# The x products of a head moved behind the projections, and its weighted sum cut into four runs

## The reference

```python
# attention, 2 x 8 heads, 768 tokens, head_dim 64, 6 hash bits
q_bits = einsum(q, proj) > 0;  k_bits = einsum(k, proj) > 0
mask = bucket(q_bits)[:, None] == bucket(k_bits)[None, :]
scores = where(mask, q @ k.T / 8, -1e9)
attn = exp(scores - max) / (sum + 1e-9)
x = (attn @ v) laid out as [1536 tokens, 512]
# experts with a capacity: a token takes its best open expert
logits = x @ w_gate                      # [1536, 8]
# greedy over all (token, expert) by falling logit, 192 tokens an expert
out[mask_e] = relu(x[mask_e] @ w1[e]) @ w2[e]
# dense layer on all tokens
h = x @ w_in;  out = (h * sigmoid(h)) @ w_out
```

## Time and profile before

| what | value |
|---|---|
| median of 3 runs | 798.89 us (794.78 to 799.8) |
| profiled execution, time | 797.15 us |
| profiled execution, span from first to last instruction | 795.4 us |
| mean granted TensorE clock | 0.99 |
| PE busy over the span | 753.1 us (95%) |
| VectorE busy | 475.0 us (60%) |
| ScalarE busy | 270.5 us (34%) |
| GpSimd busy | 155.9 us (20%) |

### The profile page before, as it was taken

How to read it: one execution, slowest core, us unless ns; L and a number is a source line. 1 busy time by engine, 2 the same in 40 slices (tenths; PEclk the granted TensorE clock), 3 DMA queues, 4 the chain that set the end, 5 groups by cost and what they waited for, 6 DMA issues and landing times.

```text
span 795.4 us, 19347 instructions
## 1 busy us (share of the span) xinstructions
PE 753.1 (95%) x7772; PEld 634.3 (80%) x7777; DVE 475.0 (60%) x1097; ACT 270.5 (34%) x551; POOL 155.9 (20%) x193
## 2 busy tenths in 40 slices
PE   8899999999998899999999999999999999999996
PEld 4577777677776658999999999988887888878885
DVE  4877777777776788977977942463333432333321
ACT  4777667766774401221222212321013111220111
POOL 5523644545434100100100100000002000020001
PEclk9999999999997999999999999999999999999999
DMA  7165354553632034534544647710001000010001
GB/s 157 35 149 126 77 136 108 126 124 80 155 105 68 23 112 142 199 147 133 187 160 133 228 144 247 264 46 1 1 0 54 0 0 0 0 53 0 0 0 53
DMA packets 58194, 75.07 MB, mean 94 GB/s; under 512 B 28736, under 2 KB 43072, under 8 KB 57120
## 3 DMA queue, kind: packets, MB, share of 16 engines
q1 hardware_dynamic: 54592, 67.12, 29.4%
q0 software_dynamic: 2208, 7.21, 2.8%
q10 hardware_dynamic: 1344, 0.04, 0.1%
HBM read 64.92 MB, written 6.29 MB: 90 GB/s over the span
## 4 chain that ended last, share of the span: by engine, by line
PE 80%; issue 8%; ACT 4%; DVE 4%; DMA 2%; POOL 1%; DVEq 0%; ACTq 0%; SPq 0%; POOLq 0%
PE quad_ps L1535 17%; PE quad_ps L1424 10%; PE quad_ps L1436 10%; PE quad_ps L1264 9%; PE score_ps L1518 8%; PE quad_ps L1518 7%; PE score_ps L1249 5%; PE score_ps L1250 3%; PE work_ps L1366 2%; ACT k_bits L531 2%; PE pv_ps L1234 2%; PE work_ps L1234 2%; DMA area<-x_rows,ids_now 1%; PE quad_ps L1273 1%; ACT att_area L537 1%
## 5 line engine op out<-in xcount | busy, mean ns | idle before, releaser
L1535 PE MATMUL quad_ps<-y_s,w_in_s 128*128 128x512 f32 x576 | 137.8, 390 | 2.7 <-DVE y_s L1171 2.0
L885 DVE TENSOR_SCALAR_CACHE_REDUCE att_area<-score_ps 128x768 f32<-128x768 f32 x96 | 91.9, 958 | 64.7 <-PE score_ps L1250 63.4
L1535 PEld LDWEIGHTS quad_ps<-y_s,w_in_s 128*128 128x128 f32 x576 | 107.9, 188 | 26.2 <-DVE y_s L1171 2.8
L1189 DVE TENSOR_TENSOR gate<-quad_ps,sig 128x512 f32<-128x512 f32 x48 | 33.2, 692 | 146.4 <-ACT sig L671 146.4
L537 ACT ACTIVATE att_area<-att_area 128x768 f32<-128x768 f32 x96 | 90.0, 938 | 75.1 <-DVE att_area L885 74.2
L671 ACT ACTIVATE sig<-quad_ps 128x512 f32<-128x512 f32 x48 | 28.7, 598 | 210.6 <-PE quad_ps L1535 210.6
L1424 PE MATMUL quad_ps<-area,experts_w 128*128 128x192 f32 x512 | 96.1, 334 | 1.5 <-ACT area L631 1.2
L1436 PE MATMUL quad_ps<-area,experts_w 128*128 128x192 f32 x512 | 87.2, 328 | 0.0
L1249 PE MATMUL score_ps<-k_parts,q_parts 128*128 128x512 f32 x192 | 73.7, 384 | 12.7 <-DVE att_area L885 11.6
L1424 PEld LDWEIGHTS quad_ps<-area,experts_w 128*128 128x128 f32 x512 | 81.8, 190 | 2.1 <-ACT area L631 2.1
L1436 PEld LDWEIGHTS quad_ps<-area,experts_w 128*128 128x128 f32 x512 | 82.9, 190 | 0.0
(11 more groups left out here) (202 smaller groups left out, 1094.2 us busy)
## 6 DMA issues: line engine op xcount, KB each, us to landing
experts_w<-in_moe_w SPq DMA_DIRECT2D x16, 2048.0 KB, 9.8
att_area<-in_v SPq DMA_DIRECT2D x64, 192.0 KB, 3.8
experts_w<-in_moe_w_in SPq DMA_DIRECT2D x8, 512.0 KB, 5.5
w_out_raw<-in_moe_w_out SPq DMA_DIRECT2D x4, 1024.0 KB, 8.9
experts_w<-in_k SPq DMA_DIRECT2D x16, 192.0 KB, 3.3
experts_w<-in_q SPq DMA_DIRECT2D x16, 192.0 KB, 3.6
k_bits<-k_parts SPq DMA_DIRECT2D x16, 192.0 KB, 3.5
x_rows<-att_area SPq DMA_DIRECT2D x8, 384.0 KB, 3.1
```

Source lines behind the costliest of these rows:

```text
L885: nc.vector.tensor_scalar(probs[c % 3], score_ps[0][:, 0:S], 0.5 * BIG, None, ALU.min, ALU.min, accum_out=neg_max[:, c:c + 1]).then_inc(s_ ...
L1189: nc.vector.tensor_tensor(gate[:, :], layer_ps[f % 2][:, 0:GT], sig[:, :], ALU.mult).then_inc(s_mul, 1)
L1535: done = nc.tensor.matmul(layer_ps[f % 2][:, 0:GT], w_in_s[:, a, w_cols], y_s[:, c, b, :], start=(c == 0 and a + b == 0), stop=(c == DC - ...
```

## The change

In the new version the x products are no fill any more. They have a semaphore of their own (`s_x_full`), a function of their own on PE (`x_rows`), and always the bank `work_ps`; they come in the third step (t = 2) of a head instead of at the end of the second. The four fills of hash bits, which stood three in the first step and one in the second, stand two and two. A fill's bank is now given by its half. The weighted sum has the shares `[4, 4, 0, 12, 4, 0]`, four runs over five steps, and its part of a step stands between the two fills of that step. The copy of the sums (`turned`) moves from t = 4 to t = 5, and VectorE's drain of x from t = 2 to t = 3. In the last pair, where steps have no fills, two matmuls of 512 columns whose product nobody reads are added in each of the steps 4 and 5 of its first head and 0 and 1 of its second. The number of matmuls that compute something is the same.

```diff
         def events(p, first, last):
-            bits = [] if last and p else [("k_bits", 0, 1), ("k_bits", 1, 1), ("q_bits", 0, 1), ("q_bits", 1, 1)]
-            x = [] if first else [("x", 0, 0)]
-            rows = [] if last else [("k", 0, 2), ("k", 1, 2), ("q", 0, 2), ("q", 1, 2)]
-            at_t = {0: bits[0:3], 1: bits[3:4] + x, 4: rows[0:2], 5: rows[2:4]}
...
+            e = {t: [] for t in range(T)}
+            if not (last and p):
+                e[0], e[1] = [("k_bits", 0, 1), ("k_bits", 1, 1)], [("q_bits", 0, 1), ("q_bits", 1, 1)]
+            if not last:
+                e[4], e[5] = [("k", 0, 2), ("k", 1, 2)], [("q", 0, 2), ("q", 1, 2)]
             return e
...
# ScalarE, pair
-                        if t == 4 and not (first and p == 0):
+                        if t == T - 1 and not (first and p == 0):
                             if not first:
-                                act.wait_ge(s_work_full, w)
+                                act.wait_ge(s_x_full, 2 * g + p - 1)
                             turned(2 * g + p - 1)
...
# VectorE, pair
-                        if t == 2 and not first:
+                        if t == 3 and not first:
                             if p == 0:
                                 dve.wait_ge(s_xw, 16 * g)
                             dve.wait_ge(s_logits, h - 1)
                             dve.wait_ge(s_norm_step, 2 * (h - 1))
-                            i = len(ev[0]) + len(ev[1]) - 1
-                            drain_x(w + i, p, bank_of(first, p, i))
+                            drain_x(h - 2, p, work_banks[0])
...
# TensorE
+            def x_rows(h, bank, free=None):
+
+                rhs = to_x[:, h % H, :] if isinstance(h, int) else to_x[:, bass.ds(h % H, 1), :].rearrange("p a e -> p (a e)")
+                if free is not None:
+                    pe.wait_ge(s_work_free, free)
+                pe.wait_ge(s_turned, h + 1)
+                for t in range(T):
+                    last = nc.tensor.matmul(bank[:, t * DE:(t + 1) * DE], weighted_t[:, t * P:(t + 1) * P], rhs, start=True, stop=True)
+                last.then_inc(s_x_full, 1)
...
-            SHARE = [0, 0, 12, 12, 0, 0]
+            SHARE = [4, 4, 0, 12, 4, 0]
...
-                        for kind, half, i, ahead in ev[t]:
-                            if kind == "x":
-                                fill_work(kind, half, u - 1, h - 2, p, bank_of(first, p, i))
-                            else:
-                                fill_work(kind, half, u if kind == "k" and half == 0 and not first else u - 1, h + ahead,
-                                          (p + ahead) % 2, bank_of(first, p, i),
-                                          x_free=h if kind == "k" and half == 1 and not first else None)
-                                u = u + 1
+                        for slot, (kind, half, ahead) in enumerate(ev[t]):
+                            if slot == 1:
+                                weighted_part(h, p, t, first, g)
+                            fill_work(kind, half, u - 1, h + ahead, (p + ahead) % 2, work_banks[half],
+                                      x_free=h if kind == "k" and half == 0 and not first else None)
+                            u = u + 1
+                        if t == 2 and not first:
+                            x_rows(h - 2, work_banks[0], u - 1)
                         if last and p == 1 and t == T - 2:
                             row_of_first_batch(u)
-                        if not (first and p == 0):
-                            weighted(h - 1, 1 - p, sum(SHARE[0:t]), SHARE[t], g if p else g - 1)
+                        if len(ev[t]) < 2:
+                            weighted_part(h, p, t, first, g)
+                        if last and (p == 0 and t >= T - 2 or p == 1 and t < 2):
+                            keep_busy(2, work_banks[1])
```

More of the change, by code:

```diff
@@ L248, in routed_layers @@
         s_halves = sem("halves_ready")
+        s_x_full = sem("x_ready")
         s_x_free = sem("x_drained")
@@ L385, in k_drained @@
             return PREP * h + 2
-        def bank_of(first, p, i):
-            return work_banks[(i + (p == 1 and not first)) % 2]
         def scatter(pool, G):
@@ L520, in _, with drain_work @@
             nc.scalar.activation(q_nat[0][:, :, 0:D].bitcast(f32r), q_nat[0][:, :, D:P], ACT.Copy).then_inc(s_first_high, 1)
-            def drain_work(kind, half, w, p_next, bank):
+            def drain_work(kind, half, w, p_next):
+                bank = first_banks[w % 4] if isinstance(w, int) and w < PREP else work_banks[half]
                 cols = slice(half * HALF, (half + 1) * HALF)
@@ L550, in _ @@
                 for half in range(2):
-                    i = PREP + 2 * t + half
-                    drain_work("q" if t else "k", half, i, 1, work_banks[i % 2])
+                    drain_work("q" if t else "k", half, PREP + 2 * t + half, 1)
             act.wait_ge(s_halves, 5)
@@ L570, in pair @@
                         n = 2 * T * g + c
-                        if t == 4 and not (first and p == 0):
+                        if t == T - 1 and not (first and p == 0):
                             if not first:
-                                act.wait_ge(s_work_full, w)
+                                act.wait_ge(s_x_full, 2 * g + p - 1)
                             turned(2 * g + p - 1)
-                        for slot, (kind, half_, i, ahead) in enumerate(ev[t]):
+                        for slot, (kind, half_, ahead) in enumerate(ev[t]):
                             if slot == 1:
                                 next_exp(n, c, last)
-                            if kind != "x":
-                                drain_work(kind, half_, w, (p + ahead) % 2, bank_of(first, p, i))
+                            drain_work(kind, half_, w, (p + ahead) % 2)
                             w = w + 1
@@ L959, in pair @@
             def pair(g, first, last):
-                w = work_base(g)
                 for p in range(2):
                     h = 2 * g + p
-                    ev = events(p, first, last)
                     for t in range(T):
@@ L983, in pair @@
                             dve.wait_ge(s_norm_step, 2 * (h - 1))
-                            i = len(ev[0]) + len(ev[1]) - 1
-                            drain_x(w + i, p, bank_of(first, p, i))
-                    w = w + sum(len(ev[t]) for t in range(T))
+                            drain_x(h - 2, p, work_banks[0])
             pair(0, True, False)
@@ L1229, in fill_work @@
                                             start=False, stop=True)
-                else:
-                    rhs = to_x[:, h % H, :] if isinstance(h, int) else to_x[:, bass.ds(h % H, 1), :].rearrange("p a e -> p (a e)")
-                    pe.wait_ge(s_turned, h + 1)
-                    for t in range(T):
-                        last = nc.tensor.matmul(bank[:, t * DE:(t + 1) * DE], weighted_t[:, t * P:(t + 1) * P], rhs,
-                                                start=True, stop=True)
-                last.then_inc(s_work_full, 1)
+                last.then_inc(s_work_full, 1)
+            def x_rows(h, bank, free=None):
[6 more added lines that the diff above has]
+                last.then_inc(s_x_full, 1)
             def scores(c, h, n, crossed):
```

33 lines of the change are left out of this document (13 added, 20 removed).

## The result

| | before | after |
|---|---|---|
| median | 798.76 us (794.78 to 799.8, 4 runs) | 776.67 us (773.34 to 778.48, 4 runs) |
| profiled execution, time and span | 797.15, 795.4 us | 777.72, 775.9 us |

The ratio is 0.9728, with an interval of 0.9679 to 0.9776: 2.7% faster.

The account below looks back on a forecast made before the run. PE's uneven load was taken as the bound: some steps overfull, others at the ring's 2.02 us. Gains of 16.8 (twelve heads), 0.5 (heads 0 and 1) and 4.6 (last pair, net) sum to 21.9, giving 776 us, range 771 to 781.

Parts of the forecast that it names:

- The prices of PE's work: PE's cost per piece, from its starts: score tile 0.70 to 0.81 us, x products 1.35, four blocks 0.93 with following cost.
- The 12 heads: Heads 2 to 13: each 1.40 us shorter, 14.44 us by its six steps, so 16.8 us in all.
- rival 1: ScalarE's copy and drains, 0.4 us margin at step 0's second bits fill, become PE's wait: 782 us; chance 0.10.
- Where the gain lies: In a head: blocks move from long steps to steps with idle PE, and a run precedes the fill that waited.
- The ring's 2.0: One score buffer: VectorE reads it 0.96 us, PE refills it 1.0, plus hand-overs; a step takes at least 2.02 us.
- The last pair: Head 14 to the last score tile: clock stays up (4.1 us), 26.90 becomes 20.9, 6.0 less; net 4.6 after the end's loss.
- The tail: Last score tile to the x products: four blocks behind the turned row, then the copy; 4.90 becomes 6.3, 1.4 us lost.
- Heads 0 and 1: The first two heads, without x products: a gain set at 0.5 us for both, between 0 and 1.4.
- rival 4: Loads become the bound: k or q land late, PE waits in step 4 of every second head; 802 at 15 us; chance 0.04.
- GpSimd's waits stay under 1 us: Sign that the loads are not the bound: GpSimd waits less than 1 us for k and q.
- the 11.2 allowed: Time from the start of v's loads to GpSimd getting k: 11.2 us allowed, 10.6 before the change, 0.6 to spare.

Follow-up runs that it names:

- the run with the blocks in one: The changed kernel with the last head's sixteen blocks, before in two runs (twelve and four), in one run in its fourth step: 776.79 us.
- the kernel with five runs: The changed kernel with the shares 4, 4, 0, 8, 4, 4, the last run in step 5 between the fills of q: 782.73 us.
- the two-input form: The changed kernel with VectorE's small operation on the row sums (adds 1e-9) written with two tensor inputs, same result: 777.04 us.

## Why the prediction held, point by point

The forecast was a gain of 21.9 us from the profiled execution. The medians lie 22.1 apart, the spans of the two profiled executions 19.5. The parts missed by 2.3, 0.5, 0.7 and 0.3 us, the largest because the clock fell in head 0 of one execution and not of the other. So the mechanism and its size held; that the median came within a microsecond is in part luck.

- **The prices of PE's work** held. A run of four was set at 0.93 with the way in; 0.10 in and 0.83 out are measured. Forecast steps of 2.53, 2.42, 2.05, 3.01, 2.46 and 1.97 stand against 2.53, 2.43, 1.96, 3.00, 2.37 and 2.00. The x products cost 1.26 (109.83 to 111.09) and not 1.35; they no longer follow a pause, and a first matmul behind one took 0.11 more; step 4's run and fill cost 0.1 less.
- **The 12 heads** gave 16.3 for 16.8, by two errors that nearly cancel. At 14.29 a head they would give 18.6. The odd heads gave back 1.9 of it (1.0 in head 5, 0.2 in each of four others) with VectorE's hold, which the prediction did not have, and head 2 another 0.4, where GpSimd waited 2.2 us for k.
- **ScalarE's drains** (rival 1, margin 0.4) never showed as a wait of PE. The run between the fills is what hides them: with it behind the fills PE stands 0.29 us in step 0, and with no run there 0.5 to 0.6 us in each of two steps.
- **Where the gain lies** was half seen. The prediction put it down to a more even load of PE, and saw one such wait filled, ahead of the x products. But by its own prices steps 0 and 1 of the kernel before hold 1.8 and 2.4 us of PE's work (a score tile and three fills; a score tile, a fill and x) and took 2.44 and 3.32: about 1.5 us of these "full" steps were waits and the pauses around them. By the same way of summing, the new placement with the old shares should take 15.3 a head, and takes 15.81; the missing 0.5 are the two drains (2.24 and 2.26 instead of 2.0 each). The ring's 2.0 holds for a step with two fills only if the drains are not late.
- **The last pair.** Its clock was sized at 4.1, and 3.8 are measured by the unread products in the old kernel. That the clock stays up was right; that unread products are needed for it was not. The four steps with unread products take 2.02 to 2.07, where three were set at 2.24 and one at 1.97.
- **The tail** lost 1.1 us up to the x products (1.4 forecast), and the run with the blocks in one did not settle whether the blocks or ScalarE's order have it. The other 0.5 us lie between the x products and the dense layer (258.99 us before, 259.54 after); the dense layer takes 270.7 to 270.8 in every profile. That stretch goes with the clock: 257.6 to 258.4 us in the three profiles without a fall in it, 259.0 in the kernel before with 3.4 us at 1.2 GHz, 259.5 to 260.4 in the eight with 6.8, the changed kernel among them, and 260.7 in the two with 10.2. So these 0.5 us need no cause in the change.
- **Heads 0 and 1**, +0.5 forecast and -1.3 measured: the clock fell in head 0 of the profiled execution. Three executions with the same work in head 0 and no fall had it at 12.68 to 12.70, against 13.04 before. In two of them heads 0 and 1 together took 26.97 and 27.00 us against 27.57, so 0.6 less: there the forecast was right.
- **The loads** (rival 4) cost no more than that 0.4 in head 2, though the sign "GpSimd's waits stay under 1 us" failed twice (2.2 in head 2, 1.1 in head 4). In head 2 GpSimd got k 11.50 us behind the start of v's loads, 0.3 over the 11.2 allowed, and the head is 0.4 longer; in head 4 it was 10.4, and nothing was lost. With the end of the sum a step later, in the kernel with five runs, the margin is used up: PE waits for GpSimd's k five times.

## What to carry to other kernels

Look for the places where the bounding engine waits between two of its own instructions, and put movable work exactly there: here twelve blocks cost 2.26 us as one run and 0.80 in three short ones, and neither the new places nor the new shares gained anything alone. After such a change, look for small instructions that have become long: a new order moves the helpers against each other. And before moving an instruction past another, list who waits for its semaphore.

## What the hardware showed

- A VectorE instruction on 128 x 6 values in SBUF, 0.13 us by itself, took 0.87 to 2.10 us when it came due during GpSimd's subtraction of 128 x 1024, and always ended within 0.04 us of its end. In the profiles of all kernels here 48 records are of that kind, six of them with the two-input form; none of the other records of this line is longer than 0.2 us.
- Going into a run of quarter-array matmuls costs 0.10 us, and coming out 0.16 (0.83 less four blocks of 0.168). A run of four may still be had for 0.2 to 0.5 us where PE would wait anyway.
- Whether the clock falls in head 0 differs between executions with the same instructions there, and shifts the whole by 0.8 to 2.0 us (13.5 to 14.7 us for the head against 12.7); falls in the stretch of the routing and the experts shift it by up to 3.1 (257.6 to 260.7). A gain below that is to be read from the starts of the score tiles in the loop, not from one time of the whole.
